# Four whole fp32 products of one weight tile multiplied as twelve split products, four ahead of an attention burst and eight behind it

## The reference

```python
for t in range(S):
    cur = einsum('bhd,bhe->bhde', u * kt, vt)
    y[:, :, t] = einsum('bhd,bhde->bhe', rt, state + cur)
    state = w * state + einsum('bhd,bhe->bhde', kt, vt)
```

## Time and profile before

| | us |
|---|---|
| median of 3 runs | 791.63 (791.34 to 792.43) |
| the profiled execution | 792.66 |
| its span, first to last instruction | 791.2 |
| PE busy in the span | 784.6 |

### The profile page before, as it was taken

The page is one execution under the profiler, slowest core; times in us unless marked ns, Lnnn a source line. Parts: engine busy times, 40 slices in busy tenths (PEclk is TensorE's granted clock), DMA queues, the critical chain, the costliest instruction groups (busy, mean ns, idle before and its releaser), DMA issues.

```text
span 791.2 us, 15799 instructions
## 1 busy us (share of the span) xinstructions
PE 784.6 (99%) x6500; PEld 677.2 (86%) x6500; DVE 429.4 (54%) x639; ACT 376.4 (48%) x647; POOL 345.8 (44%) x279
## 2 busy tenths in 40 slices
PE   8999999999999999999999999999999999999998
PEld 6999999888999888998888888888888888888886
DVE  7998655543644433123289555546555554554553
ACT  4634222222222222224367667656665765665664
POOL 2646766556566553111234335334333432433432
PEclk9999999999999999999999999999999999999999
DMA  8775445342344320202221010000001001001001
GB/s 335 267 244 149 114 145 152 91 137 85 105 139 144 89 88 22 80 0 73 68 80 41 2 41 0 1 8 33 1 1 40 1 1 40 1 1 39 2 1 40
DMA packets 47595, 57.32 MB, mean 72 GB/s; under 512 B 21794, under 2 KB 34211, under 8 KB 47523
## 3 DMA queue, kind: packets, MB, share of 16 engines
q1 hardware_dynamic: 34898, 45.83, 17.9%
q10 hardware_dynamic: 12624, 10.49, 4.3%
HBM read 46.86 MB, written 9.44 MB: 71 GB/s over the span
## 4 chain that ended last, share of the span: by engine, by line
PE 96%; DVE 3%; issue 1%; ACT 0%; POOL 0%; DVEq 0%; POOLq 0%
PE p_h L1164 25%; PE p_acc L1164 13%; PE p_a L1164 13%; PE p_b L1164 13%; PE p_out L1385 8%; PE p_out L1381 8%; PE p_out L1382 8%; PE p_s L1188 2%; PE p_y L1200 1%; PE p_y L1204 1%; PE p_acc L1313 1%; PE p_kv L1192 1%; DVE w3t_l L982 1%; PE p_b L1320 0%; PE p_acc L1299 0%
## 5 line engine op out<-in xcount | busy, mean ns | idle before, releaser
L626 POOL TENSOR_TENSOR g_l<-g,g_h 128x512 fp32r<-128x512 f32 x96 | 149.9, 1561 | 241.6 <-ACT g_h L814 241.6
L1113 DVE TENSOR_TENSOR g<-angle,p_h 128x512 f32<-128x512 f32 x96 | 65.8, 686 | 109.1 <-ACT angle L823 109.1
L490 POOL TENSOR_TENSOR g_l<-g,g_h 128x384 fp32r<-128x384 f32 (+1 forms) x56 | 70.2, 1253 | 121.0 <-ACT g_h L663 121.0
L1381 PE MATMUL p_out<-g_h,wq_l 128*128 128x512 f32 x288 | 112.1, 389 | 0.0
L1164 PE MATMUL p_h<-y_l,wi_h 128*128 128x512 f32 x288 | 112.1, 389 | 0.0
L1164 PE MATMUL p_h<-y_h,wi_h 128*128 128x512 f32 x288 | 112.1, 389 | 0.0
L1164 PE MATMUL p_h<-y_h,wi_l 128*128 128x512 f32 x288 | 112.1, 389 | 0.0
L1382 PE MATMUL p_out<-g_h,wq_h 128*128 128x512 f32 x288 | 112.0, 389 | 0.0
L814 ACT CAST g_h<-g 128x512 fp32r<-128x512 f32 x96 | 59.7, 621 | 67.5 <-PE p_out L1385 42.3
L658 ACT COPY g<-p_a 128x384 f32<-128x384 f32 (+1 forms) x56 | 29.4, 526 | 119.1 <-PE p_a L1164 117.5
L819 ACT ACTIVATE angle<-angle 128x512 f32<-128x512 f32 x96 | 60.6, 631 | 49.6 <-DVE angle L1123 49.6
(11 more groups left out here) (118 smaller groups left out, 1642.2 us busy)
## 6 DMA issues: line engine op xcount, KB each, us to landing
krT_raw<-in_kr_dims SPq DMA_DIRECT2D x24, 512.0 KB, 4.1
kr_raw<-in_kr_tokens SPq DMA_DIRECT2D x24, 384.0 KB, 4.7
v_raw<-in_v_tokens SPq DMA_DIRECT2D x24, 192.0 KB, 4.8
x_raw<-y_transposed SPq DMA_DIRECT2D x24, 192.0 KB, 2.5
out<-out_sb SPq DMA_DIRECT2D x17, 256.0 KB, 2.0
stage_b<-in_moe_w_in SPq DMA_DIRECT2D x8, 384.0 KB, 3.1
stage_b<-in_moe_w_out SPq DMA_DIRECT2D x8, 384.0 KB, 3.0
y_transposed<-yT ACTq DMA_DIRECT2D x24, 96.0 KB, 2.6
```

The costliest lines, as they stand in the source:

```text
L490: nc.gpsimd.tensor_tensor(g1_l[:, n % 2, cols], g1[:, n % 2, cols], g1_h[:, n % 2, cols].bitcast(F32), ALU.subtract).then_inc(s_gl, 1)
L626: nc.gpsimd.tensor_tensor(g2_l[:, par, :], g2[:, par, :], g2_h[:, par, :].bitcast(F32), ALU.subtract).then_inc(s_g2l, 1)
L1113: nc.vector.tensor_tensor(g2[:, n % 2, :], angle[:, n % 2, :], p_h[n % 4][:, :], ALU.mult).then_inc(s_g2, 1)
L1381: mm(bank[t][:, :], wq_l[:, f, cols], g2_h[:, f % 2, :], start=f == 0, stop=False)
```

## The change

The blocks `t` = 4 to 7 of tile 1 are no longer multiplied in whole fp32. ACT copies the high part of this half of `w3_raw` right behind `k_table` (`half_high`), and DVE subtracts the low part right behind `piece(3)` (`half_low`). PE runs the four whole products of tile 0 for `t` = 4 to 7 alone, then the four high by high products of the half, then the first burst, then four high by low and four low by high. The signal that tile 0 is done comes before the half, the one for tile 1 behind it. The wait for all low parts of `w_out` moves from tile 2 to the half.

```diff
@@ -260,6 +260,7 @@
     s_stb = [sem(f"piece_b_loaded{i}") for i in range(3)]
     s_bh, s_bl = sem("piece_b_high"), sem("piece_b_low")
     s_wth, s_wtl = sem("w3t_high"), sem("w3t_low")
+    s_half_h, s_half_l = sem("second_w3_tile_high"), sem("second_w3_tile_low")
     s_w34, s_w34h, s_w34l = sem("w34_done"), sem("w34_high"), sem("w34_low")
     s_a = sem("a_done")
     s_acp = sem("a_copied")
@@ -701,6 +702,11 @@
                 act.wait_ge(s_w34, ft - 1)
             nc.scalar.copy(w3t_h[:, ft % 2, :, :], w3_loaded_tile(ft)).then_inc(s_wth, 1)
 
+        def half_high():
+
+            act.wait_ge(s_first3[1][1], 16)
+            nc.scalar.copy(w3t_h[:, 1, NF // 2:, :], w3_raw[:, 1, NF // 2:, :]).then_inc(s_half_h, 1)
+
         def w34_high(ft):
             act.wait_ge(s_w34, ft + 1)
             nc.scalar.copy(w34_h[:, ft, :], p_acc[ft % 2][:, 0:DM]).then_inc(s_w34h, 1)
@@ -730,6 +736,7 @@
             piece(i)
         act.wait_ge(s_tabT, 1)
         nc.scalar.copy(k_table[:, :, :], p_a[:, :].rearrange("p (h e) -> p h e", e=HEAD)[:, :, 0:D]).then_inc(s_tab, 1)
+        half_high()
         w34_high(0)
         start_w3(4)
         w3t_high(2)
@@ -982,6 +989,11 @@
             nc.vector.tensor_tensor(w3t_l[:, ft % 2, :, :], w3_loaded_tile(ft),
                                     w3t_h[:, ft % 2, :, :].bitcast(F32), ALU.subtract).then_inc(s_wtl, 1)
 
+        def half_low():
+            dve.wait_ge(s_half_h, 1)
+            nc.vector.tensor_tensor(w3t_l[:, 1, NF // 2:, :], w3_raw[:, 1, NF // 2:, :],
+                                    w3t_h[:, 1, NF // 2:, :].bitcast(F32), ALU.subtract).then_inc(s_half_l, 1)
+
         def w34_low(ft):
             dve.wait_ge(s_w34h, ft + 1)
             nc.vector.tensor_tensor(w34_l[:, ft, :], p_acc[ft % 2][:, 0:DM], w34_h[:, ft, :].bitcast(F32),
@@ -1024,6 +1036,7 @@
         scale_k_dims(0)
         scale_r_dims(0)
         piece(3)
+        half_low()
         w34_low(0)
         w3t_low(2)
         sum_kur(0)
@@ -1296,7 +1309,8 @@
                 down(n)
 
         def w34_highs(ft, t):
-            return mm(p_acc[ft % 2][:, 0:DM], w3t_h[:, ft % 2, t, :], wo_h[:, t, :], start=t == 0, stop=False)
+            return mm(p_acc[ft % 2][:, 0:DM], w3t_h[:, ft % 2, t, :], wo_h[:, t, :],
+                      start=ft >= WHOLE and t == 0, stop=False)
 
         def w34_high_low(ft, t):
             return mm(p_acc[ft % 2][:, 0:DM], w3t_h[:, ft % 2, t, :], wo_l[:, t, :], start=False, stop=False)
@@ -1311,7 +1325,7 @@
             if t % 2 == 0:
                 pe.wait_ge(s_st[t // 2], 16)
             return mm(p_acc[ft][:, 0:DM], w3_raw[:, ft, t, :], A_SLOTS[t // 2][:, t % 2 * DM:(t % 2 + 1) * DM],
-                      start=t == 0, stop=t == NF - 1)
+                      start=t == 0, stop=ft == 0 and t == NF - 1)
 
         pe.wait_ge(s_S0, 1)
         zeros = state[:, :, :, :].rearrange("p c h e -> p (c h e)")
@@ -1319,11 +1333,11 @@
         for _ in range(WARM):
             mm(p_b[:, 0:2 * P], zeros[:, 0:P], zeros[:, 0:2 * P], start=True, stop=True)
         for i in range(NWO):
-            for ft in range(WHOLE):
+            for ft in range(WHOLE if i < NWO // 2 else 1):
                 for t in (2 * i, 2 * i + 1):
                     ins = w34_whole(ft, t)
-                if i == NWO - 1:
-                    ins.then_inc(s_w34, 1)
+            if i == NWO - 1:
+                ins.then_inc(s_w34, 1)
             if i == 1:
                 pe.wait_ge(s_pairs, 2)
                 pe.wait_ge(s_masks, 2)
@@ -1331,7 +1345,18 @@
                     ins = nc.tensor.transpose(p_a[:, hp * P:(hp + 1) * P],
                                               k_pairs[:, hp, :, :].rearrange("p s t -> p (s t)"), ident[:, :])
                 ins.then_inc(s_tabT, 1)
+        pe.wait_ge(s_half_h, 1)
+        pe.wait_ge(s_sth, NWO)
+        for t in range(NF // 2, NF):
+            w34_highs(1, t)
         first_burst()
+        pe.wait_ge(s_stl, NWO)
+        for t in range(NF // 2, NF):
+            w34_high_low(1, t)
+        pe.wait_ge(s_half_l, 1)
+        for t in range(NF // 2, NF):
+            ins = w34_low_high(1, t)
+        ins.then_inc(s_w34, 1)
         for f in range(WHOLE, NF):
             pe.wait_ge(s_wth, f - WHOLE + 1)
             pe.wait_ge(s_w34l, f - 1)
@@ -1339,8 +1364,6 @@
                 w34_highs(f, t)
             if f == WHOLE + 1:
                 burst(1, 0)
-            if f == WHOLE:
-                pe.wait_ge(s_stl, NWO)
             for t in range(NF):
                 w34_high_low(f, t)
             if WHOLE + 2 <= f <= WHOLE + HC:
```

## The result

Over eleven runs of each, the changed kernel takes 793.72 us (792.26 to 794.38) and the kernel before 792.12 (791.34 to 793.43). The ratio on record is 1.0016, with a 95% interval of 1.0009 to 1.0024 (it is not the quotient of the two medians, which is 1.0020). The profiled execution of the changed kernel took 793.67 us, with a span of 792.1.

The account below looks back on a forecast made before the run. PE and DVE chains side by side were taken to bound the kernel up to tile 6. PE's 0.48 us saving ends in waits for DVE, whose lateness is absorbed to 0 to 0.1: likeliest 791.6 us, range 790.4 to 792.7.

Parts of the forecast that it names:

- The bound: Up to tile 6, PE's and DVE's chains run side by side, DVE's ending 0.67 us later at most; gains need both.
- PE's saving: Four whole blocks go (2.58 us), twelve split products come (2.10): 0.48 us less on PE, ending in waits for DVE.
- The turns of DVE and POOL: From `half_low` to `decayed`, one waits until the other's instruction is over; `half_low` ends at 17.1, `z` begins at 19.15.
- The loss: DVE 0.45 us late at `z` of the first chunk; absorbed by `decayed`, leaving 0 to 0.1 us.
- Case 3: DVE asks 0.1 later at 21.82, POOL goes first, DVE waits about 0.85 us: 792.5; chance 0.18.
- ACT and the transfers: w3 tile 4 issued about 1.3 us sooner, tiles 5 and 6 about 0.5 later; costed at nothing, bounds nothing and 0.6.
- the cover: POOL's waits at 19.34 and 25.56 for `kr` to land hide the shifts; gone if either landing comes later.

Follow-up runs that it names:

- the last: Kernel before with the whole products' order changed, w3 tile 4 issued later and eight tiny matmuls behind the warm-up; ratio 1.0019, tile 6 at 45.27.
- `kr` first: SP issues `kr` of the second chunk ahead of w3 tile 3 and `krT`; on the kernel before: first `k_sc` to tile 6 28.53 us, ratio 1.0002.
- the operations alone: Kernel before plus `half_high` and `half_low`, whose output nothing reads, PE in the old order; ratio 1.0000, first `k_sc` to tile 6 29.15 us.
- the later transfer: Changed kernel with ACT issuing the transfer of w3 tile 4 behind the cast of tile 2, not ahead of it; ratio 1.0001, then 1.0011.
- Order alone: Kernel before with only the order of whole products changed: tile 0 blocks 4 to 7, then tile 1's; no half operations; ratios 1.0003 and 1.0005.

## Why the prediction was wrong

**The bound** was read rightly. Tile 6 starts when DVE has emptied its bank, in every kernel of the table but the last, where the pause comes in between. That the landing of `kr` is what DVE's chain hangs on was read rightly too: with `kr` first the kernel before is 0.61 shorter there.

**PE's saving** came as worked out: tile 2 at 17.94 against a forecast 17.87, the second burst at 23.89 against 24.05 (the high products were recorded from 14.24, forecast 14.59). It ended in PE's waits of 0.9, 0.6 and 0.3 us.

**The turns of DVE and POOL** were right in kind and a little too dark. `half_low` took 1.49 (forecast: due at 15.6, held to 16.47 and through at 17.1; measured: 15.53 to 17.02); `z` started at 18.91, not 19.15. The loss was absorbed, and the kernel with the operations alone shows it with PE's work and the transfers left as they were. Case 3, a turn lost at 21.8, did not happen: DVE's product there took 0.67 again.

**The step that failed** is the one on ACT and the transfers: "I cost these at nothing, since what POOL waits for at 19.34 and 25.56 is named as `kr`, and the first of these was issued ahead of all that moves". I took the order of issue for the order of service; between two queues it was not. The transfers' cost was bounded by nothing and 0.6, and the likeliest time was worked out with nothing; it measures 0.91 at the landing and 0.97 at tile 6, and five kernels with the later transfer or without the earlier signal come back to 29.1. The same paragraph named the condition, "the cover is gone if either landing comes later than its row", but gave it no case of its own. The case of 792.5 (0.85 us) has about the size of this term and another cause. On 791.63, a ratio of 1.0016 is 792.9, and the upper end of the range was 792.7; this term alone would give 792.6, so the number left the range only with the second one. That the change would stay under 0.2% held, at 0.16% (0.09 to 0.24).

The Trainium skill, page "DMA: Bandwidth & Descriptors", section "Queues, rings and completion order", says that each transfer engine takes turns between the queues that have work, packet by packet. The trace of the changed kernel agrees once the later transfer is under way: from 18.2 us to the landing of `kr` ACT's queue moves 0.48 MB and SP's 0.35 (shown in the last section). By that rule the earlier issue had to cost SP's queue something.

**What the prediction did not have at all** is the pause near 95 us. It was in the trace of before with 0.46, and I read nothing of that stretch, as no instruction of the change lies there: the words were "From there to the end there is PE work almost without a break". Together the two terms are 0.97 and about 0.6 (0.68 less 0.07) against 1.3 us timed (1.0016) and 1.4 (1.0018). With the transfer later, the changed kernel keeps 0.0006, the mean of two measurements (1.0001, 1.0011). Order alone, with the first term and without the second, has 0.0004, again the mean of two, and 0.9996 when its transfer is later as well. That 0.0004 is under the 0.0011 of its stretches, and no run here says why; each of the two intervals just reaches it.

**What stays open.** What PE waits for at the pause. The traces mark some transfers as instruction; in the execution with 1.16 shown, three of them start near there, at 90.3, 94.8 and 98.1 us, the middle one with 16 KB (94.7 to 94.8 us):

```profile
q8 instruction: 1, 0.02, 54.9%
```

Such a transfer starts ahead of the 1348th record in all sixteen traces that have this record next to the burst near 95 us. In the nine with a pause, PE goes on 2.2 to 2.5 us behind its start; in the seven without, the record starts 2.2 to 2.9 behind it, and in none sooner than that. That fits instructions that come late, but it is a reading: no run here held them back by themselves. With intervals some 0.001 to either side, the second term is better seen in the traces than in the times.

## What to carry to other kernels

A signal that fires sooner starts whatever waits for it, transfers included. List each transfer whose wait ends sooner and ask which earlier transfers of other queues are still under way, and who waits for them. Here one signal 1.3 us sooner cost 0.97 us at tile 6, and moving the issue by one place in the list took that back. A saving on the busiest engine is worth nothing while another chain sets its next start; and where the effect is a tenth of a per cent, compare whole traces by their distances from the end before naming one cause.

## What was not expected of the hardware

A transfer issued by ACT while SP's queue had work moved nothing for about 3.5 us, and then took about half of the bytes (0.38 to 0.58 of them up to the landing of `kr`, in the five traces of the changed kernel and of order alone). Issued at 14.74 in the changed kernel, it has moved nothing up to 18.2 us, where only q1 is listed (14.74 to 18.2):

```profile
q1 hardware_dynamic: 450, 1.42, 101.2%
```

From 18.2 to the landing of `kr` at 20.18 both are there:

```profile
q10 hardware_dynamic: 122, 0.48, 58.9%
q1 hardware_dynamic: 153, 0.35, 44.2%
```

Issued at 16.09 in the kernel before, it shows none up to 19.4 (above), just after `kr` had landed at 19.27. The kernel before thus missed this meeting by about 0.1 us. In the seventeen traces the first packet comes 2.9 to 3.5 us behind the issue, but 1.8 behind it in the kernel that issues at 18.7.

And PE can pause with nothing named as its releaser, here for up to 1.5 us near 95 us and for 1.7 once near 43. With four more matmul records at the start the pause near 95 us was there in seven of eight executions, without them in two of eight, which makes work added at the start felt 80 us later.
